# Turning the first mixer's residual with VectorE's block transposes and transfers

## The chip, the cores and the metric

The kernel runs on one core of a Trainium2 chip. Its metric is the device time in microseconds (us). The engines are TensorE (PE; its weight loads are listed as PEld), VectorE (DVE), ScalarE (ACT), GpSimd (POOL) and SyncE (SP), which issues all transfers. They run side by side and meet at semaphores.

## The reference

Attention over 8 heads with a local window and a few global keys gives `x` of 2 x 768 x 512 (batch, tokens, channels). Two mixers follow. The change lies in the first one:

```python
xt = x.transpose(0, 2, 1)
h = np.maximum(xt @ w_tok1, 0.0) @ w_tok2      # over tokens: 768 -> 256 -> 768
u = x + h.transpose(0, 2, 1)
h2 = np.maximum(u @ w_ch1, 0.0) @ w_ch2        # over channels: 512 -> 1536 -> 512
x = u + h2
```

The second mixer (angles, sine and cosine, token products, channel product) follows on its output. All is in fp32.

## The kernel before

Every fp32 matrix product is made of three products of parts: each operand is split into a rounded high part (`hi`, fp32r) and the rest (`lo`), and `three` (line 272 holds its matmul) issues hi x hi, hi x lo and lo x hi. The matmuls of both mixers up to the last channel product have this one line. ScalarE usually makes the high part, VectorE the low part; of the weights, GpSimd makes both (lines 573 and 574), chunk by chunk of 1536 columns, in one buffer pair `wraw` that SP fills (line 432).

Attention works in 48 steps (12 tiles of 128 tokens, 4 pairs of heads each). In a step VectorE takes the scores from PSUM (line 903), splits keys and queries of a later step (lines 810 and 799), and divides the weighed values into `act_raw`, where a tile lies with tokens on partitions (line 829). GpSimd splits queries (506) and, between them, the first two weight chunks. Eight more chunks follow behind the last tile of batch 0.

The first mixer, for each batch b: `hidden_tokens` gives 2 x 128 hidden units with the 512 channels as columns in banks 4 and 5; ScalarE and VectorE make high and low parts in `hid` (717, 1007). `mixed_tokens(s, j)` gives `h` for 128 tokens on partitions and 512 channels as columns, 6 tiles of 2 x 3 matmuls. VectorE adds the rows of `act_raw` into `u_rows` (1024), `turn_u` turns them on TensorE with four transposes into bank 4 or 5 (1243), and ScalarE (723) and VectorE (1016, from the bank) make the parts of the turned `u` in `split`, channels on partitions and tokens as columns. `hidden` and `reduce_hidden` then work in 24 blocks (2 halves of 384 tokens, 12 blocks of 128 hidden units), 12 matmuls each. In order: hidden 0, the last `turn_u`, hidden 1, reduce 0, hidden 2, reduce 1 and so on; the relu's parts are made by ScalarE (732) and VectorE (1034), and reduce i waits for the low part of block i.

The order of work on each engine is the order of its program, written out by hand; there is no planner. On VectorE the additions and low parts of `u` alternate, and the low part of hidden block 0 stands behind them. GpSimd's first chunk after attention waits for the last tile of batch 0 to be split (`tile_lo`), the chunk of the second mixer's first weights for all of `h` of batch 1 (`h_ready`). SP's list is: queries, keys and values of all tiles, two weight chunks between them, then the other weights, each behind `w_ready`, then the outputs.

Of the kernel before, what the change touches and what calls it, by code (L numbers as in the profile page):

```python
# [27 lines left out]
P = 128  # L28
# [42 lines left out]
HALF = 1024  # L71
BORROWED = 5
# [13 lines left out]
def build(nc, qk, v, both_counts, weights, out):  # L86
# [11 lines left out]
    with ctx:  # L98

        probs_mem = ExitStack()  # L100
# [4 lines left out]
        wraw = sb("wraw", [P, 2, CHUNK])  # L105
        act_raw = sb("act_raw", [P, B, DM * S // P])
# [56 lines left out]
        u_rows = sb("u_rows", [P, 2, DM], F32, mix1_mem)  # L163
# [55 lines left out]
        uT_ready = sem("uT_ready")  # L219
# [69 lines left out]

        def load_flag(eng):  # L290
            eng.wait_ge(flag_ready, 1)
            return eng.value_load(use_general[0:1, 0:1], min_val=0, max_val=1)

        def general_sync(sp, flag):
            with sp.If(flag > 0):
                sp.wait_ge(x_done, 2 * UNITS)
                for b, h, t, c in general_tiles(sp):
                    sp.wait_ge(gen_x, c + 1)
                    sp.dma_start(g_q[:, :], qk[b, bass.ds(t, 1), 0:D, bass.ds(h, 1), 0:P].rearrange(
                        "t d o s -> (t d) (o s)")).then_inc(gen_in, 16)  # L300
                    sp.dma_start(g_k[:, :].rearrange("d (t s) -> d t s", t=T),
                                 qk[b, :, 0:D, bass.ds(h, 1), P + G:].rearrange(
                                     "t d o s -> d t (o s)")).then_inc(gen_in, 16)
                    sp.dma_start(g_v[:, :, :], v[b, :, :, 0, bass.ds(h * VD, D)].rearrange(
                        "t s d -> s t d")).then_inc(gen_in, 16)

# [32 lines left out]
        def general_vector(dve, flag):  # L339
            with dve.If(flag > 0):  # L340
# [57 lines left out]
                dve.wait_ge(gen_x, B * H * T + 1)  # L398
                for g in range(AHEAD):
# [27 lines left out]
        def _(sp):  # L427
# [42 lines left out]
        def _(pool):  # L470
# [83 lines left out]
            for i in range(len(BESIDE), len(ORDER)):  # L554
# [33 lines left out]
        def _(act):  # L588
# [121 lines left out]
            for b in range(B):  # L710
# [8 lines left out]
                for s in range(T):  # L719
                    act.wait_ge(uT_ready, b * T + s + 1)  # L720
                    if b and s == 0:
                        act.wait_ge(x2_done, b * NC * KD)
                    act.activation(split[:, 0].rearrange("p (k s) -> p k s", k=KD)[:, :, s * P:(s + 1) * P],
                                   bank[4 + s % 2][:, :].rearrange("p (k s) -> p k s", k=KD),
                                   ACT.Copy).then_inc(uT_hi, 1)
# [44 lines left out]
        def _(dve):  # L770
# [101 lines left out]
            for m in range(STEPS):  # L872
# [119 lines left out]
            for b in range(B):  # L992
# [26 lines left out]
                for s in range(T):  # L1019
                    g = b * T + s  # L1020
                    dve.wait_ge(h_ready, g + 1)
                    if g >= 2:
                        dve.wait_ge(uT_ready, g - 1)
                    dve.tensor_tensor(u_rows[:, s % 2], bank[s % 4][:, :], raw[:, s * DM:(s + 1) * DM],
                                      ALU.add).then_inc(u_done, 1)
# [84 lines left out]
        def _(pe):  # L1110
# [79 lines left out]
            def hidden_tokens(b, s, j):  # L1190
# [3 lines left out]
                if b and s == 0:  # L1194
                    pe.wait_ge(uT_lo, b * T)
# [24 lines left out]
            for b in range(B):  # L1220
# [16 lines left out]
                def turn_u(s):  # L1237
                    g = b * T + s
                    pe.wait_ge(u_done, g + 1)
                    if g >= 2:  # L1240
# [6 lines left out]
                def mixed_tokens(s, j):  # L1247
                    g = b * T + s
                    pe.wait_ge(h1_lo, b * KJ + j + 1)
                    if j == 0 and s >= 4:  # L1250
                        pe.wait_ge(u_done, g - 3)
                    if b and j == 0 and s < 4:
                        pe.wait_ge(acc_taken, ((b * NC) - 1) * KD + s + 1)
                    return three(pe, bank[s % 4][:, :], lambda a: w_at(TOK2, a, j * S + s * P, P),
                                 lambda a: h1s[:, j, a], j == 0, j == KJ - 1)

                mixed_tokens(0, 0)
                mixed_tokens(1, 0)
                for s in range(T):
                    if s >= 2:  # L1260
                        mixed_tokens(s, 0)
                    mixed_tokens(s, 1).then_inc(h_ready, 1)
                    if s >= 2:
                        turn_u(s - 2)
                turn_u(T - 2)


                def hidden(i):
# [4 lines left out]
                    if f == 0:  # L1273
                        pe.wait_ge(uT_lo, b * T + (c + 1) * T // NC)
# [8 lines left out]
                def reduce_hidden(i):  # L1283
# [4 lines left out]
                    pe.wait_ge(r1_lo, g + 1)  # L1288
                    for d in range(KD):
# [8 lines left out]
                turn_u(T - 1)  # L1298
# [134 lines left out]
```

## Time and profile before

| | |
|---|---|
| median of 3 runs | 513.64 us (513.61 to 514.79) |
| the profiled execution's own time | 514.9 us |
| its span | 512.7 us |
| TensorE's share of the chain that ended last | 91% |
| share of it in the matmuls of line 272 | 72% |
| transfers | 37.20 MB, mean 73 GB/s |

The span is what the profile covers, from the first instruction to the last; the execution's own time also holds what lies around it. The chain is followed back from the last instruction to what released it at each step. A group's line number can be that of a helper (line 272), so the names of tiles tell which product it is.

### The profile page before, as it was taken

What the parts mean: (1) busy time and instruction counts of PE and PEld (TensorE: products, weight loads), DVE (VectorE), ACT (ScalarE), POOL (GpSimd) and SP (SyncE); (2) the same over time, 40 slices, a digit from 0 to 9 for tenths busy, and PEclk for the clock granted to TensorE, in tenths of its full rate; (3) what the DMA queues carried; (4) which work ended last, traced back from release to release, by engine and by line L of the source; (5) the groups of instructions that cost most, each with busy time, mean ns of one, the idle gap of its engine ahead of it and who ended that gap; (6) DMA issues with size and microseconds to landing.
All of it is one profiled execution on the core that took longest, in us unless ns stands there. A gap on an engine that the chain in (4) does not pass through costs nothing.

```text
span 512.7 us, 8107 instructions
## 1 busy us (share of the span) xinstructions
PE 504.5 (98%) x3049; PEld 471.1 (92%) x3049; DVE 258.8 (50%) x679; ACT 173.9 (34%) x371; POOL 144.2 (28%) x143
## 2 busy tenths in 40 slices
PE   7999999999999999999999999999999999999997
PEld 5899999879999999979999999998888899888897
DVE  7999998552111421164111424166775565754452
ACT  6899898521111111122111143413322320321130
POOL 4576766199900000005000041820310310000040
PEclk9999999999999999999999999999999999999999
DMA  5886675135410000003000011420000011000002
GB/s 195 310 301 233 221 264 160 45 123 150 137 42 1 0 2 0 1 0 99 28 0 1 0 63 61 124 83 0 1 1 2 0 63 61 1 1 0 1 31 93
DMA packets 9112, 37.20 MB, mean 73 GB/s; under 512 B 1136, under 2 KB 3184, under 8 KB 7664
## 3 DMA queue, kind: packets, MB, share of 16 engines
q1 hardware_dynamic: 9072, 36.67, 21.1%
q8 instruction: 25, 0.41, 0.3%
q14 instruction: 15, 0.12, 0.1%
HBM read 33.52 MB, written 3.15 MB: 72 GB/s over the span
## 4 chain that ended last, share of the span: by engine, by line
PE 91%; DMA 3%; DVE 2%; issue 1%; POOL 1%; ACT 1%; DVEq 0%; POOLq 0%; ACTq 0%
PE bank L272 72%; PE bank L1360 7%; PE bank L1125 3%; PE bank L1155 3%; PE bank L1158 2%; DMA qk_raw<-qk 2%; PE bank L1139 1%; PE bank L1137 1%; PE bank L1216 1%; PE bank L1243 1%; POOL wsplit L506 1%; DMA counts<-both_counts 1%; PE bank L1165 0%; DVE scores L903 0%; ACT bias L618 0%
## 5 line engine op out<-in xcount | busy, mean ns | idle before, releaser
L272 PE MATMUL bank<-hid,wsplit 128*128 128x384 f32 (+1 forms) x648 | 126.4, 344 | 0.1
L272 PEld LDWEIGHTS bank<-hid,wsplit 128*128 128x128 f32 x648 | 113.2, 188 | 4.0 <-issue 0.7
L272 PE MATMUL bank<-split,wsplit 128*128 128x384 f32 x576 | 108.1, 337 | 0.0
L272 PE MATMUL bank<-wsplit,zs 128*128 128x512 f32 (+1 forms) x576 | 104.1, 340 | 0.0
L272 PEld LDWEIGHTS bank<-wsplit,zs 128*128 128x128 f32 x576 | 89.1, 188 | 13.3
L272 PEld LDWEIGHTS bank<-split,wsplit 128*128 128x128 f32 x576 | 100.3, 188 | 0.0
L1034 DVE SCALAR_TENSOR_TENSOR hid<-bank,hid 128x384 fp32r<-128x384 f32 x48 | 26.7, 557 | 140.4 <-ACT hid L732 140.4
L574 POOL TENSOR_TENSOR wsplit<-wraw,wsplit 128x1536 fp32r<-128x1536 f32 (+1 forms) x18 | 58.7, 3263 | 75.5 <-ACT wsplit L693 74.5
L732 ACT ACTIVATE hid<-bank 128x384 fp32r<-128x384 f32 x48 | 23.6, 491 | 143.4 <-PE bank L272 143.4
L573 POOL CAST wsplit<-wraw 128x1536 fp32r<-128x1536 f32 (+1 forms) x12 | 15.9, 1328 | 136.1 <-PE bank L272 122.8
L506 POOL TENSOR_TENSOR wsplit<-qk_raw,wsplit 64x256 fp32r<-64x256 f32 x48 | 38.9, 810 | 26.5 <-DVE wsplit L810 24.8
L583 POOL TENSOR_TENSOR split<-act_raw,split 128x384 fp32r<-128x384 f32 x12 | 12.5, 1069 | 113.5 <-ACT split L766 113.5
L650 ACT ACTIVATE probs<-scores,nmax 128x232 f32<-128x232 f32 (+1 forms) x96 | 39.9, 465 | 2.4 <-DVE nmax L903 2.3
L697 ACT ACTIVATE zb<-zb 128x512 f32<-128x512 f32 x12 | 7.6, 632 | 96.1 <-DVE zb L976 96.1
L272 PE MATMUL bank<-wsplit,tile 128*128 128x512 f32 x144 | 35.5, 395 | 0.0
L1125 PE MATMUL bank<-wsplit 128*128 128x232 f32 (+1 forms) x192 | 32.7, 292 | 2.5 <-DVE wsplit L799 1.2
L1155 PE MATMUL bank<-vt,probsT 128*128 128x65 f32 x192 | 33.9, 265 | 0.9 <-ACT probsT L596 0.9
L1360 PE MATMUL bank<-split,wsplit 128*128 128x384 f32 x192 | 34.6, 341 | 0.0
L903 DVE CUSTOM_DVE_ANT_0 scores<-bank,bias 128x232 f32<-128x232 f32 (+1 forms) x96 | 32.4, 373 | 3.0 <-PE bank L1125 2.7
L1360 PEld LDWEIGHTS bank<-split,wsplit 128*128 128x128 f32 x192 | 33.8, 188 | 0.0
L272 PEld LDWEIGHTS bank<-wsplit,tile 128*128 128x128 f32 x144 | 26.4, 188 | 5.5
L1158 PE MATMUL bank<-vt,probsT 104*128 104x65 f32 x160 | 30.9, 275 | 0.0
(101 smaller groups left out, 583.3 us busy)
## 6 DMA issues: line engine op xcount, KB each, us to landing
wraw<-weights SPq DMA_DIRECT2D x16, 768.0 KB, 4.2
qk_raw<-qk SPq DMA_DIRECT2D x11, 1056.0 KB, 5.5
vt<-v SPq DMA_DIRECT2D x10, 520.0 KB, 5.2
out<-act_raw SPq DMA_DIRECT2D x16, 192.0 KB, 1.9
wraw<-weights SPq DMA_DIRECT2D x4, 512.0 KB, 3.5
qk_raw<-qk SPq DMA_DIRECT2D x2, 264.0 KB, 3.5
qk_raw<-qk SPq DMA_DIRECT2D x1, 528.0 KB, 6.0
vt<-v SPq DMA_DIRECT2D x2, 260.0 KB, 6.4
```

The lines of the kernel that those rows point to most:

```text
L272: mm = pe.matmul(dst, lhs(a), rhs(c), start=first and i == 0, stop=last and i == 2, skip_group_check=True)
L506: pool.tensor_tensor(q_split[D:P, n % 2, heads], q_in[D:P, n % 2, heads], q_split[D:P, n % 2, heads].bitcast(F32), ALU.subtract).then_inc( ...
L573: link(pool.tensor_copy(w_at(slot, 0, 0, width), raw))
L574: pool.tensor_tensor(w_at(slot, 1, 0, width), raw, w_at(slot, 0, 0, width).bitcast(F32), ALU.subtract).then_inc(w_ready, 1)
L650: act.activation(probs[:, n % 2, h, first:], scores[:, m % 2, e, first:], ACT.Exp, bias=nmax[:, n % 2, h:h + 1], scale=-1.0).then_inc(exp_ ...
L732: act.activation(r1s[:, i % 3, 0], bank[6 + i % 2][:, 0:SC], ACT.Relu).then_inc(r1_hi, 1)
L903: dve.tensor_tensor_reduce(out=scores[:, m % 2, e, first:], in0=S_BANK[m % 2][e][:, first:WIN], in1=bias[:, h, first:], scale=-SCALE, scal ...
L1034: dve.scalar_tensor_tensor(r1s[:, i % 3, 1], bank[6 + i % 2][:, 0:SC], 0.0, r1s[:, i % 3, 0].bitcast(F32), ALU.max, ALU.subtract).then_inc ...
L1125: mm = pe.matmul(S_BANK[m % 2][e][:, first:WIN], q_split[:, n % 2, h, :], k_split[:, i, h, key:key + WIN - first], start=i == 0, stop=i == 1)
L1155: mm = pe.matmul(dst, probsT[:, m % 2, at + P:at + 2 * P], vt[:, n % 2, 0, cols], start=m % 2 == 0 and e == 0, stop=n % T == 0, skip_group ...
L1158: mm = pe.matmul(dst, probsT[0:SEEN, m % 2, at:at + P], vt[0:SEEN, n % 2, 1, cols], start=False, stop=True, skip_group_check=True)
L1360: return pe.matmul(bank[at][:, 0:SC], w_at(CHAN_AT[k_ // 2], w, k_ % 2 * DM + d * P, P), S_(u, k_, c * SC, SC), start=first, stop=last, sk ...
```

## The change

The residual is turned ahead of time instead of `u` behind the product. VectorE's `transpose` of a 128 x 512 tile turns its 32 x 32 blocks in place; 16 transfers between partition groups of 32 then put the blocks where they belong, so that `xT` holds `x` with channels on partitions. Batch 0's six tiles are turned in attention's steps 26, 29, ..., 41 into `turned_early`, which lies in weight slots not yet in use; batch 1's in two sets of three, behind hidden blocks 3 to 5 and 9 to 11 of batch 0. SP issues batch 0's 16 transfers behind its last load of `v` and in front of the third weight chunk, batch 1's 2 x 16 behind weight chunk 11. GpSimd's third chunk waits for `xT_in` too.

`mixed_tokens(i, j)` now takes `hid` as the stationary operand and 384 columns of the weights as the moving one: 8 blocks of 128 channels x 384 tokens. VectorE adds `xT` from SBUF to the bank and writes `u` back into `xT`; ScalarE copies the high part out of `xT`, and VectorE's `lo_of_u` subtracts that from `xT`. `turn_u` is gone. Hidden 0 waits for four low parts (`uT_lo`), reduce 0 for all eight additions (`u_done`).

```diff
+        def move_quads(sp, src, first, count, done):
+            from_ = src.rearrange("p (t q c) -> p t q c", t=count, q=P // QUAD)
+            to = xT[:, first * DM:(first + count) * DM].rearrange("p (t a c) -> p t a c", t=count, a=P // QUAD)
+            for a in range(P // QUAD):
+                for q in range(P // QUAD):
+                    sp.dma_start(to[q * QUAD:(q + 1) * QUAD, :, a],
+                                 from_[a * QUAD:(a + 1) * QUAD, :, q]).then_inc(done, 16)
+
+        def turn_rows(dve, dst, b, t):
+            return dve.transpose(dst, act_raw[:, b, t * DM:(t + 1) * DM].rearrange(
+                "p (k q i) -> p q k i", k=KD, q=P // QUAD))
...
+            sp.wait_ge(x_turned, T)
+            move_quads(sp, turned_early[:, :], 0, T, xT_in)
             general_sync(sp, load_flag(sp))
             for i in range(len(BESIDE), len(ORDER)):
                 load_weight(i)
+                if i == SLOTS + 1:
+                    for first in range(0, T, STAGED):
+                        sp.wait_ge(x_turned, T + first + STAGED)
+                        move_quads(sp, turned[:, :], first, STAGED, xT_in)
...
                     pool.wait_ge(tile_lo, T)
+                    pool.wait_ge(xT_in, BATCH_IN)
                 if i == SLOTS + THETA:
-                    pool.wait_ge(h_ready, B * T)
+                    pool.wait_ge(h_ready, B * OUTB)
...
+                for i in range(OUTB):
+                    act.wait_ge(u_done, b * OUTB + i + 1)
...
+                    act.activation(by_quads(split[:, 0, u_cols(i)]), xT_at(i), ACT.Copy).then_inc(uT_hi, 1)
...
+                t, off = divmod(m - TURN_FROM, TURN_EVERY)
+                if 0 <= t < T and off == 0:
+                    dve.wait_ge(x_done, 2 * t + 2)
+                    turn_rows(dve, turned_early[:, t * DM:(t + 1) * DM], 0, t).then_inc(x_turned, 1)
...
-                def lo_of_uT(s):
-                    dve.wait_ge(uT_hi, b * T + s + 1)
-                    dve.tensor_tensor(rows_at(lo_, s), bank[4 + s % 2][:, :].rearrange("p (k s) -> p k s", k=KD),
-                                      rows_at(hi, s).bitcast(F32), ALU.subtract).then_inc(uT_lo, 1)
...
+                def lo_of_u(i):
+                    dve.wait_ge(uT_hi, b * OUTB + i + 1)
+                    dve.tensor_tensor(by_quads(lo_[:, u_cols(i)]), xT_at(i),
+                                      by_quads(hi[:, u_cols(i)].bitcast(F32)), ALU.subtract).then_inc(uT_lo, 1)
+
+                dve.wait_ge(xT_in, (2 * b + 1) * BATCH_IN)
+                for i in range(OUTB):
+                    dve.wait_ge(h_ready, b * OUTB + i + 1)
+                    dve.tensor_tensor(xT_at(i), by_quads(U_BANK[i][:, 0:SC]), xT_at(i),
                                       ALU.add).then_inc(u_done, 1)
-                    if s:
-                        lo_of_uT(s - 1)
-                lo_of_uT(T - 1)
-                dve.wait_ge(u_done, (b + 1) * T)
+                    if i:
+                        lo_of_u(i - 1)
+                lo_of_u(OUTB - 1)
...
+                    if b == 0 and 3 <= i < 3 + 2 * T and (i - 3) % T < STAGED:
+                        t = (i - 3) // T * STAGED + (i - 3) % T
+                        if t == STAGED:
+                            dve.wait_ge(xT_in, 2 * BATCH_IN)
+                        turn_rows(dve, turned[:, t % STAGED * DM:(t % STAGED + 1) * DM], b + 1,
+                                  t).then_inc(x_turned, 1)
...
-                def turn_u(s):
-                    g = b * T + s
-                    pe.wait_ge(u_done, g + 1)
-                    if g >= 2:
-                        pe.wait_ge(uT_lo, g - 1)
-                    for d in range(KD):
-                        mm = pe.transpose(bank[4 + s % 2][:, d * P:(d + 1) * P],
-                                          u_rows[:, s % 2, d * P:(d + 1) * P], ident[:, :])
-                    mm.then_inc(uT_ready, 1)
-
...
+                def mixed_tokens(i, j):
+                    c, k_ = divmod(i, KD)
                     pe.wait_ge(h1_lo, b * KJ + j + 1)
...
+                    if j == 0 and i in (6, 7):
+                        pe.wait_ge(u_done, b * OUTB + i - 5)
...
+                    return three(pe, U_BANK[i][:, 0:SC], lambda a: h1s[:, j, a, k_ * P:(k_ + 1) * P],
+                                 lambda a: w_at(TOK2, a, j * S + c * SC, SC), j == 0, j == KJ - 1)
+
+                for i in range(KD):
+                    mixed_tokens(i, 0)
+                for i in range(KD):
+                    mixed_tokens(i, 1).then_inc(h_ready, 1)
+                for i in range(KD, OUTB):
+                    mixed_tokens(i, 0)
+                    mixed_tokens(i, 1).then_inc(h_ready, 1)
...
                     if f == 0:
-                        pe.wait_ge(uT_lo, b * T + (c + 1) * T // NC)
+                        pe.wait_ge(uT_lo, b * OUTB + (c + 1) * KD)
...
                     pe.wait_ge(r1_lo, g + 1)
+                    if i == 0:
+                        pe.wait_ge(u_done, (b + 1) * OUTB)
```

## Rows read from the trace of the kernel before

**Rows 1.** The page, busy time, share of the span and instructions of the engines.
```profile
PE 504.5 (98%) x3049; PEld 471.1 (92%) x3049; DVE 258.8 (50%) x679; ACT 173.9 (34%) x371; POOL 144.2 (28%) x143
```

**Rows 2.** The chain of waits in time's order, batch 0's mix: start, us, what.
```profile
107.89 0.44 PE bank L1243 x4
108.33 1.40 PE bank L272 x6
...
112.04 0.61 ACT split L723
...
114.02 0.66 PE bank L1243 x4
114.67 2.12 PE bank L272 x12
```

**Rows 3.** Timeline, both mixes: start, us, engine, line, operation, tiles, count, idle before.
```profile
103.46 4.44 PE L272 MATMUL bank<-hid,wsplit 128*128 128x512 f32 x18
...
119.20 1.98 PE L272 MATMUL bank<-hid,wsplit 128*128 128x384 f32 x10
...
223.64 4.48 PE L272 MATMUL bank<-hid,wsplit 128*128 128x512 f32 x18
...
239.39 1.79 PE L272 MATMUL bank<-hid,wsplit 128*128 128x384 f32 x9
```

**Rows 4.** Windows: stretch, length, each engine's busy time, TensorE's clock, transfers.
```profile
7.00:9.00 2.00, 0.83 (x5) 0.40 (x4) 1.86 (x7) 1.49 (x7) 0.73 (x1) 1.00 0.99 410
...
54.00:60.00 6.00, 5.49 (x50) 5.37 (x49) 5.97 (x28) 4.78 (x15) 4.63 (x7) 1.00 0.78 272
...
66.00:72.00 6.00, 6.00 (x56) 6.00 (x56) 5.70 (x30) 5.92 (x16) 4.68 (x8) 1.00 0.74 263
```

**Rows 5.** Timeline, attention.
```profile
1.45 5.16 PE L1165 MATMUL bank<-wsplit 128*128 128x512 f32 x13 [1.45 <-DVE wsplit L779]
...
59.09 0.68 PE L1125 MATMUL bank<-wsplit 128*128 128x232 f32 x4 [0.52 <-DVE nmax L903]
...
63.05 0.52 POOL L533 CAST wsplit<-wraw 128x256 fp32r<-128x256 f32 x1
...
63.32 0.54 DVE L799 TENSOR_TENSOR wsplit<-qk_raw,wsplit 128x272 fp32r<-128x272 f32 x1
```

**Rows 6.** Timeline, GpSimd's weights beside batch 0's mix.
```profile
100.70 1.47 POOL L573 CAST wsplit<-wraw 128x1536 fp32r<-128x1536 f32 x1 [13.28 <-DVE third L860]
...
102.25 3.51 POOL L574 TENSOR_TENSOR wsplit<-wraw,wsplit 128x1536 fp32r<-128x1536 f32 x1
...
105.71 1.47 POOL L573 CAST wsplit<-wraw 128x1536 fp32r<-128x1536 f32 x1
```

**Rows 7.** Timeline, VectorE on two SBUF tiles of 384 columns, GpSimd idle.
```profile
341.66 1.96 DVE L957 TENSOR_TENSOR act_raw<-act_raw,split 128x384 f32<-128x384 f32 x4
```

**Rows 8.** Timeline, VectorE beside a subtraction of GpSimd in the second mixer.
```profile
358.20 0.69 DVE L984 TENSOR_TENSOR zc<-bank,zc 128x512 f32<-128x512 f32 x1 [1.31 <-ACT zc L698]
...
359.00 2.41 POOL L574 TENSOR_TENSOR wsplit<-wraw,wsplit 128x1024 fp32r<-128x1024 f32 x1
...
359.59 2.37 DVE L989 TENSOR_TENSOR zs<-zc,zs 128x512 fp32r<-128x512 f32 x1
...
361.88 0.68 DVE L989 TENSOR_TENSOR zs<-zb,zs 128x512 fp32r<-128x512 f32 x1
```

**Rows 9.** Timeline, GpSimd at the end of batch 1's mix.
```profile
233.77 1.04 POOL L573 CAST wsplit<-wraw 128x1024 fp32r<-128x1024 f32 x1 [93.06 <-PE bank L272]
```

**Rows 10.** Timeline, SP at the end of attention.
```profile
82.41 0.33 SPq L455 DMA_DIRECT2D vt<-v  x1
83.79 3.98 SPq L432 DMA_DIRECT2D wraw<-weights  x2
```

**Rows 11.** The page, transfers: tiles, queue, count, KB each, us to landing.
```profile
wraw<-weights SPq DMA_DIRECT2D x16, 768.0 KB, 4.2
...
out<-act_raw SPq DMA_DIRECT2D x16, 192.0 KB, 1.9
```

More of the change, by code:

```diff
@@ L71 @@
 HALF = 1024
+QUAD = 32
+TURN_FROM = 26
+TURN_EVERY = 3
+STAGED = 3
+BATCH_IN = 16 * 16
 BORROWED = 5
@@ L98, in build @@
     with ctx:
+        turned_mem = ExitStack()
+        sb("below_turned", [P, CH1, 2, CHUNK], F32, turned_mem)
+        turned_early = sb("turned_early", [P, T * DM], F32, turned_mem)
+        turned_mem.close()
         probs_mem = ExitStack()
@@ L105, in build @@
         wraw = sb("wraw", [P, 2, CHUNK])
+        xT = sb("xT", [P, DM * S // P])
         act_raw = sb("act_raw", [P, B, DM * S // P])
@@ L162, in build @@
         zc = sb("zc", [P, DM])
-        u_rows = sb("u_rows", [P, 2, DM], F32, mix1_mem)
+        turned = sb("turned", [P, STAGED * DM], F32, mix1_mem)
         hid = sb("hid", [P, 2 * 3 * SC], F32R, mix1_mem)
@@ L218, in build @@
         u_done = sem("u_done")
-        uT_ready = sem("uT_ready")
+        x_turned = sem("x_turned")
+        xT_in = sem("xT_in")
+        gen_turned = sem("gen_turned")
+        gen_xT = sem("gen_xT")
         uT_hi = sem("uT_hi")
@@ L284, in build, with xT_at, by_quads, u_cols @@
         U2_DVE = [(0, d) for d in range(2, KD)]
+        U_BANK = [bank[0], bank[1], bank[2], bank[3], bank[4], bank[5], bank[0], bank[1]]
+        def xT_at(i):
+            c, k_ = divmod(i, KD)
+            groups = SC // QUAD
+            return xT[:, :].rearrange("p (w k j) -> p k w j", k=KD, j=QUAD)[:, k_, c * groups:(c + 1) * groups]
+        def by_quads(ap):
+            return ap.rearrange("p (w j) -> p w j", j=QUAD)
+        def u_cols(i):
+            c, k_ = divmod(i, KD)
+            return slice(k_ * S + c * SC, k_ * S + (c + 1) * SC)
+        def move_quads(sp, src, first, count, done):
[8 more added lines that the diff above has]
+                "p (k q i) -> p q k i", k=KD, q=P // QUAD))
         def load_flag(eng):
@@ L305, in general_sync @@
                         "t s d -> s t d")).then_inc(gen_in, 16)
+                sp.wait_ge(gen_turned, T)
+                move_quads(sp, turned_early[:, :], 0, T, gen_xT)
         def general_pool(pool, flag):
@@ L398, in general_vector @@
                 dve.wait_ge(gen_x, B * H * T + 1)
+                dve.wait_ge(xT_in, BATCH_IN)
+                for t in range(T):
+                    turn_rows(dve, turned_early[:, t * DM:(t + 1) * DM], 0, t).then_inc(gen_turned, 1)
+                dve.wait_ge(gen_xT, BATCH_IN)
                 for g in range(AHEAD):
@@ L717, in _ @@
                     act.activation(h1s[:, j, 0], bank[4 + j][:, :], ACT.Relu).then_inc(h1_hi, 1)
-                for s in range(T):
-                    act.wait_ge(uT_ready, b * T + s + 1)
-                    if b and s == 0:
+                for i in range(OUTB):
+                    act.wait_ge(u_done, b * OUTB + i + 1)
+                    if b and i == 0:
                         act.wait_ge(x2_done, b * NC * KD)
-                    act.activation(split[:, 0].rearrange("p (k s) -> p k s", k=KD)[:, :, s * P:(s + 1) * P],
-                                   bank[4 + s % 2][:, :].rearrange("p (k s) -> p k s", k=KD),
-                                   ACT.Copy).then_inc(uT_hi, 1)
+                    act.activation(by_quads(split[:, 0, u_cols(i)]), xT_at(i), ACT.Copy).then_inc(uT_hi, 1)
                 for i in range(CHB):
@@ L1194, in hidden_tokens @@
                 if b and s == 0:
-                    pe.wait_ge(uT_lo, b * T)
+                    pe.wait_ge(u_done, b * OUTB)
                 return three(pe, bank[4 + j][:, :], lambda a: w_at(TOK1, a, s * F_TOK + j * P, P),
@@ L1257, in _ @@
[L1257 to L1265, printed above, removed]
+                def mixed_tokens(i, j):
+                    c, k_ = divmod(i, KD)
+                    pe.wait_ge(h1_lo, b * KJ + j + 1)
+                    if j == 0 and i in (4, 5):
+                        pe.wait_ge(h1_lo, (b + 1) * KJ)
+                    if j == 0 and i in (6, 7):
+                        pe.wait_ge(u_done, b * OUTB + i - 5)
+                    if b and j == 0 and i < KD:
+                        pe.wait_ge(acc_taken, ((b * NC) - 1) * KD + i + 1)
+                    return three(pe, U_BANK[i][:, 0:SC], lambda a: h1s[:, j, a, k_ * P:(k_ + 1) * P],
+                                 lambda a: w_at(TOK2, a, j * S + c * SC, SC), j == 0, j == KJ - 1)
@@ L1297, in _ @@
                 hidden(0)
-                turn_u(T - 1)
                 for i in range(1, CHB):
@@ L1425 @@
     }
-    nc = bacc.Bacc("TRN2", target_bir_lowering=False, num_devices=1)
+    nc = bacc.Bacc("TRN2", target_bir_lowering=False, num_devices=1,
+                   dynamic_dma_scratch_size=1024)
     args = [nc.dram_tensor(n, a.shape, mybir.dt.from_np(a.dtype), kind="ExternalInput").ap()
```

14 lines of the change are left out of this document (removed).

## The prediction

> **What bounds the kernel now.** First the page: TensorE is busy 98% of the span, VectorE half of it, GpSimd 28% [rows 1]. Then the chain of waits in order of time: behind attention it is TensorE's own matmuls, with short breaks [rows 2]. So a change pays only by taking work or a break from TensorE, and costs only where another engine makes TensorE wait. In the token mixer the chain shows what could go: groups of four transposes at 0.44 us, and one visit to ScalarE, an issue and VectorE before the next group. The same stretch as a timeline gives its length: the second token product starts at 103.46 and the first product that needs `hid` again at 119.20, 15.74 us; in batch 1 223.64 to 239.39, 15.75 [rows 3]. I call these two stretches the mixes. Next I read who is near its limit beside TensorE: in attention VectorE is busy 5.97 of 6 us in the stretch from 54 [rows 4] and once makes TensorE wait 0.52 [rows 5]; GpSimd works without a break from 100.70, splitting eight chunks of weights [rows 6], which is exactly while batch 0's mix runs.
>
> **TensorE's own sum.** Removed: 12 groups of transposes, 12 x 0.44 = 5.3 us, 2.65 a mix. The token product keeps its columns: before 36 matmuls of 512, after 48 of 384. Six of 512 take 1.40 (0.233 each), twelve of 384 take 2.12 (0.177 each) [rows 2]; 8.40 becomes 8.50. Two hidden products are 24 x 0.177 = 4.25. Before: 8.40 + 2.65 + 4.25 = 15.3, so 0.44 of the 15.74 is breaks, and the chain's 112.04 to 114.02 is where they stand. After, if nothing is late: 8.50 + 4.25 = 12.75, 2.99 less a mix, 6.0 in all. This is what the edit can give.
>
> **Who feeds the hidden product now.** Per 384-column block VectorE adds the residual and later subtracts ScalarE's rounded copy. Before, both operations read one PSUM operand; now the add reads PSUM and `xT`, but the subtraction (`lo_of_u`) reads `xT` and `split`, both in SBUF. An operation of 384 columns of either kind takes 0.55 and follows the last after 0.49 (four in 1.96) [rows 7], so a block costs VectorE 0.98 and TensorE 6 x 0.177 = 1.06. Undisturbed, the fourth subtraction ends some 0.9 us before TensorE finishes block 8: no wait, and `xT` is ready as below.
>
> **GpSimd beside it.** A VectorE operation with two SBUF inputs does not run beside GpSimd's. At 359.00 GpSimd starts a subtraction of 2.41 us; VectorE's add from PSUM at 358.20, beside GpSimd's cast, takes its usual 0.69, but the subtraction of two SBUF tiles at 359.59, otherwise 0.69, takes 2.37, to 0.55 past GpSimd's end; the next starts at 361.88, 0.47 past it [rows 8]. The pair of rows comes once more in the trace, a tile later, and attention has the same on a small scale. GpSimd's casts hold VectorE too: one from 63.05 to 63.57, and a VectorE subtraction with two SBUF inputs that starts inside it at 63.32 ends at 63.86 [rows 5]. So VectorE waits for the GpSimd instruction in progress and goes before the next. GpSimd alternates 1.55 (cast) and 3.46 us (subtraction), start to start [rows 6].
> The Trainium skill, SBUF — State Buffer, section "SBUF: two separate sides", says it as an exclusive lock held for a whole instruction, also for two SBUF inputs against a GpSimd operation that reads SBUF. It adds what no row shows, that an operation with one SBUF input outside the two-port modes is free of it; by that the six new transposes are not stopped, and the sum below has nothing for them; if they were, each would wait for up to one GpSimd slice, and the attention term would go towards its upper bound.
>
> **Batch 0, step by step** (clock of the profile before). Mix starts 103.46; blocks are ready at 106.1, 106.6, 107.2, 107.7, then each 1.06 later. Add 0 at 106.4; ScalarE's copy ends 107.5; subtraction 0 is asked at 107.5 and waits for GpSimd's 107.25-110.7. Then add 2, subtraction 1 waits for the cast (till 112.6), add 3, subtraction 2 waits for the next 3.46 (till 116.6), add 4, subtraction 3 till 118.5. It alternates: subtractions 4 to 7 start at 122.4, 124.4, 128.3, 130.3. A pair takes 1.5 + 3.5 + twice 0.47. TensorE has ended its 48 matmuls at 111.97, waits for subtraction 3 until 119.3, does hidden 0 and 1 to 123.5, and then waits again: VectorE makes the low part of hidden 0 only behind subtraction 7, at 131.2, so the reduction starts at 131.4. Before it started at 119.20: 12.2 us lost. Shifting GpSimd's phase by -1.5 to +4.5 us in the same steps gives 9.7 to 12.2; if subtraction 7 keeps its place right behind 6, 1.4 less.
> TensorE's clock: granted 1.00, and its longest break is the 1.2 us in the stretch from 7 to 9 [rows 4]; now it idles 7 and 8 us. The kernel's first 13 matmuls of 512 columns, after idling, took 5.16 us [rows 5]; at 0.233 each 13 take 3.03 [rows 2]. I charge one such start, 2.1 us, behind the second wait (the first one's is covered). Bounds 0 and 4.2.
> The Trainium skill, TensorE: Matmul & The Clock Gate, Part 1, says that an idle engine returns to half of 2.4 GHz, which is the direction of this term; that the granted clock reads 1.00 in those first microseconds as well is not explained by it.
>
> **Batch 1.** GpSimd idles 93 us until all of `h` is done and then, from 233.77, runs 1.04 [rows 9], 2.41 [rows 8] and both once more. Subtractions 0 to 4 or 5 are through; two or three are held, the reduction starts at 238.0 to 238.9 instead of 236.4. Against 239.39 this is 0.5 to 1.4 gained; I take 1.4 (bounds 0.5 and 3.0).
>
> **Attention.** Six transposes of 128x512 are added to VectorE. No row shows one; the nearest is a 512-column VectorE operation, 0.69 [rows 8]; below it stands 0.49, the pace of 384 columns [rows 7], above it twice 0.69, if the blocks went through in two passes. The first stands at step 26, near 56 us, where VectorE has no idle time [rows 4] and TensorE already waits for it [rows 5]: 0.65 in full. The other five add 3.45 in the next 27 us, of which VectorE's idle 0.3 in 6 us (5.70 busy, from 66) takes back 1.3 [rows 4]. The 2.1 left are a lag, and two sets of scores cover one step of it (16 matmuls of 56 in 6 us, 1.7 us [rows 4]): some 0.5 reaches TensorE. I take 1.2. Bounds: 0, if the buffers take all, and 6 x 0.69 = 4.1.
> The Trainium skill, VectorE: DVE Perf Modes, section "The three transpose paths", gives 311 ns for 128x128 in bf16 on VectorE; four make 1.24 us by estimate, nearly twice my 0.69, and would make the attention term about 4 us.
>
> **SP, the transfers and the weights.** On SP weight 2 is issued at 83.79, right behind the last load of `v` [rows 10]. The 16 moves go ahead of it. An issue takes 0.33 [rows 10]: 5.3 us of SP, so weight 2 starts near 89. A transfer of 768 KB lands in 4.2, one of 192 KB in 1.9 [rows 11]; 16 moves of 98 KB at the first's rate end near 93, all one behind the other at 1.9 each at 114. I take 96. GpSimd first needs `xT` at 100.70 [rows 6], VectorE at 106.4 as above, and GpSimd weight 2 at 100.70, so this costs nothing; if late, GpSimd's chain shifts, which is in the phases above. Weight 2 is split by 105.7 [rows 6] and used at 114.67 [rows 2], the next one five later and at 119.20 [rows 3]: 8.5 us of cover, and the need comes later now. Batch 1's transposes and moves stand at hidden blocks 3 to 5 and 9 to 11, 4.25 us each with 1.1 us of VectorE work, on a queue with no load due: nothing. Should GpSimd stop such a transpose for 3.5 us, the next low part would be 0.5 late against some 0.8 of cover.
>
> **Sum.** +12.2 + 2.1 - 1.4 + 1.2 = +14.1 us. The profiled execution has a span of 512.7 and its own time is 514.9, 1.3 above the median 513.64. It would take 529.0; against the median 527.7.
>
> **Rivals.**
> (a) No hold-up in the mixes (faster). If VectorE's subtractions slip through, the change gives its 6.0 less 1.2 of attention: 508.8. For it: the sum of matmuls is certain. Against it: the stretched operations of rows 8. It decides at one place, the duration of `lo_of_u` beside GpSimd: 0.55 or up to 4. Undisturbed, the reduction would start at 116.2; from 3 us of holds on, less than one GpSimd subtraction, batch 0's mix is slower than before, and from 8 us on the whole kernel.
> (b) GpSimd goes first after each of its instructions. As it has no gaps, subtraction 0 waits for the end of the eighth chunk, 100.7 + 8 x 5.0 = 140.7; seven more blocks follow, the reduction starts near 149: about 545. Against it: in rows 8 VectorE goes on right behind GpSimd, though there GpSimd had nothing next.
> (c) Moves at 1.9 us each: `xT` at 114, first add 7.6 us later, then the same alternation: 535. For it: pieces of 32 partitions that no row shows. Against it: 768 KB that land in 4.2 [rows 11].
>
> **Chances.** Forecast 0.80, its own range 521 to 534 (phase and slot -3.9, clock -2.1 and +2.1, attention -1.2 and +2.9, batch 1 -1.6 and +0.9; not all on one side). (a) 0.12, (b) 0.03, (c) 0.05. Were casts no hindrance and only GpSimd's subtractions held VectorE, a pair would take 5.5 instead of 5.9 us and the result would stay in this range. The range 517 to 536 leaves out (a), (b) and some of the forecast's own edges. A change of 0.3% (1.5 us) is about what can be told from none. Faster: (a), 0.11; within: 0.01 of (a) and 0.01 of the forecast; slower: 0.87.
>
> **What would show it.** Right: in batch 0's mix `split<-xT,split` on VectorE with a mean of 2 to 3 us, each ending 0.55 after a GpSimd instruction, and TensorE waiting about 7 and 8 us for VectorE; the same operation at 0.55 in batch 1's first blocks; TensorE waits in attention of about 1 us in all. Wrong: `lo_of_u` at 0.55 throughout in batch 0, or a transpose that takes well over 0.7, or GpSimd waiting for a transfer beyond 100.70.

## The result, and the profile after

The changed kernel takes 526.99 us (median of 6 runs, 524.45 to 528.58); the kernel before took 514.7 in the same session (513.61 to 515.26). The ratio is 1.024, interval 1.021 to 1.027: slower, as forecast (527.7). The two profiled executions compared below have spans of 526.8 and 512.7 us, so 14.1 us have to be found.

The page of the changed kernel: busy time of the engines, and two lines of the span in 40 slices.

```profile
PE 506.8 (96%) x3025; PEld 476.6 (90%) x3025; DVE 282.1 (54%) x699; ACT 175.1 (33%) x375; POOL 147.0 (28%) x143
...
PE   8999999955999999999999999999999999999997
...
PEclk9999999997899999999999999999999999999999
```

Against [rows 1] TensorE has 24 instructions fewer but is busy 2.3 us longer (a slower clock, below), and VectorE is busy 23.3 us longer for 20 instructions more. The slices put the place at the ninth and tenth, 105 to 132 us, batch 0's first mixer. The matmuls of line 285 are those of line 272 before. TensorE's waits, all of them in us, times, longest:

```profile
PE bank L285 <- DVE split L1070: 6.4, 1, 6.4
PE bank L285 <- DVE hid L1085: 6.1, 2, 5.2
```

VectorE in batch 0's mix (start, us, engine, line, operation, tiles, shape, count). L1076 adds `xT` to the bank, L1070 is `lo_of_u`:

```profile
107.36 1.02 DVE L1076 TENSOR_TENSOR xT<-bank,xT 128x384 f32<-128x384 f32 x2 [1.73 <-PE bank L285]
108.52 3.62 DVE L1070 TENSOR_TENSOR split<-xT,split 128x384 fp32r<-128x384 f32 x1
112.06 0.54 DVE L1076 TENSOR_TENSOR xT<-bank,xT 128x384 f32<-128x384 f32 x1
112.53 1.35 DVE L1070 TENSOR_TENSOR split<-xT,split 128x384 fp32r<-128x384 f32 x1
113.80 0.55 DVE L1076 TENSOR_TENSOR xT<-bank,xT 128x384 f32<-128x384 f32 x1
114.27 3.31 DVE L1070 TENSOR_TENSOR split<-xT,split 128x384 fp32r<-128x384 f32 x1
...
125.17 5.06 DVE L1070 TENSOR_TENSOR split<-xT,split 128x384 fp32r<-128x384 f32 x2
130.16 1.01 DVE L1085 SCALAR_TENSOR_TENSOR hid<-bank,hid 128x384 fp32r<-128x384 f32 x2
```

The pair from 125.17 in the view of its tile, over that stretch alone (ns, shortest, median, longest, then the first and last start):

```profile
L1070 DVE TENSOR_TENSOR split<-xT,split x2: 1812/2570/3327, 125.2 to 128.4; 128x384 fp32r<-128x384 f32 x2
```

GpSimd beside it:

```profile
108.22 3.51 POOL L626 TENSOR_TENSOR wsplit<-wraw,wsplit 128x1536 fp32r<-128x1536 f32 x1
111.66 1.81 POOL L625 CAST wsplit<-wraw 128x1536 fp32r<-128x1536 f32 x1
113.55 3.61 POOL L626 TENSOR_TENSOR wsplit<-wraw,wsplit 128x1536 fp32r<-128x1536 f32 x1
117.11 1.79 POOL L625 CAST wsplit<-wraw 128x1536 fp32r<-128x1536 f32 x1
...
128.03 1.79 POOL L625 CAST wsplit<-wraw 128x1536 fp32r<-128x1536 f32 x1
```

Two things show here. The addition, with one operand in PSUM, keeps 0.54 us; it starts at 112.06 beside GpSimd's cast and is not held. The subtractions, with both in SBUF, end at 112.14, 113.88 and 117.58, each 0.41 or 0.42 behind the end of the GpSimd instruction beside it (111.73, 113.47, 117.16). And the hold works both ways: GpSimd's cast, 1.47 us before [rows 6], takes 1.81 where a VectorE subtraction goes first. The two engines alternate, one instruction each, even where VectorE has no addition between: of the last two subtractions the first (3.33) waits for GpSimd's subtraction and the second (1.81) for its cast at 128.03. TensorE over the same stretch:

```profile
104.37 8.71 PE L285 MATMUL bank<-wsplit,hid 128*128 128x384 f32 x48
119.46 6.17 PE L285 MATMUL bank<-split,wsplit 128*128 128x384 f32 x24 [6.38 <-DVE split L1070]
130.80 4.18 PE L285 MATMUL bank<-hid,wsplit 128*128 128x384 f32 x12 [5.18 <-DVE hid L1085]
134.78 3.26 PE L285 MATMUL bank<-split,wsplit 128*128 128x384 f32 x12
137.88 2.28 PE L285 MATMUL bank<-hid,wsplit 128*128 128x384 f32 x12
```

The clock in windows (stretch, length, busy time and count of PE, PEld, DVE, ACT, POOL, then the granted clock, transfers):

```profile
116.00:119.40 3.40, 0.00 (x0) 0.00 (x0) 3.40 (x4) 0.53 (x1) 3.32 (x3) 0.57 0.37 103
119.40:126.00 6.60, 6.17 (x24) 5.88 (x24) 6.60 (x6) 1.77 (x4) 6.52 (x3) 0.71 0.51 183
...
130.80:134.00 3.20, 3.20 (x10) 3.20 (x11) 0.36 (x1) 0.00 (x0) 3.20 (x2) 0.50 0.17 71
134.00:137.80 3.80, 3.80 (x16) 3.80 (x15) 0.00 (x0) 0.00 (x0) 3.72 (x2) 0.61 0.65 211
137.80:141.00 3.20, 3.20 (x20) 3.20 (x19) 0.56 (x1) 0.49 (x1) 3.12 (x3) 1.00 0.45 137
```

Behind each stop TensorE runs at 0.50, the 1.2 GHz level, and returns to 1.00 while it works. In windows of 0.2 us the granted clock is 0.50 from 116.5 to 123.3, and again from 130.1 to 136.9; of the first of these stretches 3.8 us lie behind the restart at 119.46, of the second 6.1 us behind the restart at 130.80.

Batch 1's mix, where GpSimd comes late (TensorE, then VectorE, then GpSimd):

```profile
239.82 8.74 PE L285 MATMUL bank<-wsplit,hid 128*128 128x384 f32 x48
248.40 4.40 PE L285 MATMUL bank<-split,wsplit 128*128 128x384 f32 x24
253.73 2.37 PE L285 MATMUL bank<-hid,wsplit 128*128 128x384 f32 x12 [0.93 <-DVE hid L1085]
```
```profile
248.66 0.55 DVE L1070 TENSOR_TENSOR split<-xT,split 128x384 fp32r<-128x384 f32 x1
...
249.59 3.61 DVE L1070 TENSOR_TENSOR split<-xT,split 128x384 fp32r<-128x384 f32 x2
```
```profile
248.70 1.42 POOL L625 CAST wsplit<-wraw 128x1024 fp32r<-128x1024 f32 x1 [105.20 <-PE bank L285]
250.20 2.59 POOL L626 TENSOR_TENSOR wsplit<-wraw,wsplit 128x1024 fp32r<-128x1024 f32 x1
```

The same `lo_of_u` takes 0.55 while GpSimd idles, and the last two of eight are held together.

The moves and transposes (from the page, KB each and us to landing; from the tile's own view, ns min/median/max; from SP's timeline):

```profile
xT<-turned_early SPq DMA_DIRECT2D x16, 96.0 KB, 2.6
```
```profile
L322 SPq DMA_DIRECT2D xT<-turned_early x16: 590/614/872, 83.7 to 94.1; - x16
L326 DVE STREAM_TRANSPOSE turned_early<-act_raw x6: 697/698/704, 56.3 to 82.7; 128x512 f32<-128x512 f32 x6
```
```profile
83.70 11.03 SPq L322 DMA_DIRECT2D xT<-turned_early  x16
96.42 0.81 SPq L477 DMA_DIRECT2D wraw<-weights  x2
```

Where the 14.1 us are, from these rows and [rows 3]:

| stretch | before | after | difference |
|---|---|---|---|
| start of the kernel to batch 0's mix | 103.46 | 104.37 | +0.9 |
| batch 0's mix to its first reduction | 15.74 | 26.43 | +10.7 |
| that reduction to batch 1's mix | 104.44 | 109.02 | +4.6 |
| batch 1's mix to its first reduction | 15.75 | 13.91 | -1.8 |
| the rest | 273.3 | 273.1 | -0.2 |

The third line has two parts. The first 24 matmuls of 384 columns after the second stop take 7.08 us (130.80 to 137.88); at the pace of the blocks before, 4.16 for 24, that is +2.9. The remaining +1.7 I had no cause for: 21 later blocks take 4.24 us each instead of 4.16. VectorE's low part of the relu comes once a block and shows it, before and after:

```profile
140.80 0.56 DVE L1034 SCALAR_TENSOR_TENSOR hid<-bank,hid 128x384 fp32r<-128x384 f32 x1 [3.60 <-ACT hid L732]
144.96 0.56 DVE L1034 SCALAR_TENSOR_TENSOR hid<-bank,hid 128x384 fp32r<-128x384 f32 x1 [3.60 <-ACT hid L732]
```
```profile
147.09 0.56 DVE L1085 SCALAR_TENSOR_TENSOR hid<-bank,hid 128x384 fp32r<-128x384 f32 x1 [3.07 <-ACT hid L782]
...
151.32 0.56 DVE L1085 SCALAR_TENSOR_TENSOR hid<-bank,hid 128x384 fp32r<-128x384 f32 x1 [3.06 <-ACT hid L782]
```

The starts are 4.16 and then 4.23 apart, with the granted clock at 1.00 in both. In batch 1 the changed kernel is back at 4.16 behind its stop of 0.93.

### The profile page after: what moved, and what is told of

Read it like the earlier page. It is cut to its first block, busy times and chain, and to the rows that moved or that the text cites. A ratio compares the mean times of both kernels' runs of the same rounds, so it can differ in the third digit from the quotient of the medians.

```text
span 526.8 us, 8116 instructions
## 1 busy us (share of the span) xinstructions
PE 506.8 (96%) x3025; PEld 476.6 (90%) x3025; DVE 282.1 (54%) x699; ACT 175.1 (33%) x375; POOL 147.0 (28%) x143
## 4 chain that ended last, share of the span: by engine, by line
PE 86%; DVE 8%; DMA 3%; POOL 1%; ACT 1%; issue 1%; DVEq 0%; POOLq 0%; ACTq 0%
PE bank L285 67%; PE bank L1408 6%; DVE split L1070 5%; PE bank L1182 3%; PE bank L1212 3%; PE bank L1215 2%; DMA qk_raw<-qk 2%; PE bank L1196 1%; DVE xT L1076 1%; PE bank L1194 1%; PE bank L1273 1%; POOL wsplit L557 1%; DMA counts<-both_counts 1%; PE bank L1222 0%; ACT bias L670 0%
## 5 line engine op out<-in xcount | busy, mean ns | idle before, releaser
L285 PE MATMUL bank<-split,wsplit 128*128 128x384 f32 x576 | 111.2, 344 | 6.4 <-DVE split L1070 6.4
L285 PE MATMUL bank<-hid,wsplit 128*128 128x384 f32 x576 | 110.4, 342 | 6.1 <-DVE hid L1085 6.1
L285 PEld LDWEIGHTS bank<-split,wsplit 128*128 128x128 f32 x576 | 104.2, 193 | 6.7 <-issue 6.7
L285 PEld LDWEIGHTS bank<-hid,wsplit 128*128 128x128 f32 x576 | 102.9, 191 | 6.8 <-issue 5.5
L625 POOL CAST wsplit<-wraw 128x1536 fp32r<-128x1536 f32 (+1 forms) x12 | 17.9, 1493 | 146.8 <-PE bank L285 134.3
L1408 PE MATMUL bank<-split,wsplit 128*128 128x384 f32 x192 | 34.3, 339 | 0.0
L1408 PEld LDWEIGHTS bank<-split,wsplit 128*128 128x128 f32 x192 | 33.5, 188 | 0.0
```

The costliest lines, as they stand in the source:

```text
L285: mm = pe.matmul(dst, lhs(a), rhs(c), start=first and i == 0, stop=last and i == 2, skip_group_check=True)
L1408: return pe.matmul(bank[at][:, 0:SC], w_at(CHAN_AT[k_ // 2], w, k_ % 2 * DM + d * P, P), S_(u, k_, c * SC, SC), start=first, stop=last, sk ...
```

## The experiments

By the prediction two facts together make the hold-up: `lo_of_u` has two operands in SBUF, and GpSimd works at the same time. The first two runs take away one each. The rival is that something else (the idle itself, the moves, the transposes) makes the time. Each run's time is a median with its own median of the kernel before; ratios have their 95% interval.

**u_in_bank.** The sum is written back to the bank, and ScalarE and VectorE read it there; GpSimd is left as it is.

```diff
-  dve.tensor_tensor(xT_at(i), by_quads(U_BANK[i][:, 0:SC]), xT_at(i), ALU.add)
+  dve.tensor_tensor(by_quads(U_BANK[i][:, 0:SC]), by_quads(U_BANK[i][:, 0:SC]), xT_at(i), ALU.add)
   # lo_of_u and ScalarE's copy: xT_at(i) -> by_quads(U_BANK[i][:, 0:SC])
   # TensorE's three waits for u_done -> the same counts of uT_lo
```

> The changed kernel, but VectorE's addition writes u back into its PSUM bank (ScalarE's copy and VectorE's subtraction read the bank), so the subtraction has one SBUF input as before the change. Theory (GpSimd's weight instructions hold VectorE's operations with two SBUF inputs): subtractions take 0.55 us in batch 0 as well, the mix falls from 26.4 to about 12.8 us, TensorE never idles there, no slow clock: about 527 - 13.7 (mix) - 4.6 (clock and pace behind it) - 1 (batch 1) = 508 us against 514.7 before. Rival (the subtraction is slow for its access pattern, or because the transfers into xT are late): it stays stretched or the first addition stays late, 520 us or more.

Measured: 512.2 us against 514.55, ratio 0.995 (0.994 to 0.997). VectorE, then GpSimd:

```profile
108.44 0.56 DVE L1071 TENSOR_TENSOR split<-bank,split 128x384 fp32r<-128x384 f32 x1
```
```profile
108.16 3.51 POOL L626 TENSOR_TENSOR wsplit<-wraw,wsplit 128x1536 fp32r<-128x1536 f32 x1
111.62 1.46 POOL L625 CAST wsplit<-wraw 128x1536 fp32r<-128x1536 f32 x1
```

Beside the same GpSimd subtraction the operation now takes 0.55 instead of 3.62, GpSimd's cast is back at 1.46, and neither mix has a stop. The sum kept in PSUM, where VectorE's subtraction and with it ScalarE's copy read it, is worth 14.8 us against the changed kernel (526.99 to 512.2). It misses the expected 508 by 4: all blocks of batch 0 and the first 17 of batch 1 now take 4.24 us, 40 x 0.08 = 3.2 us; the last six of batch 1 take 4.16.

**gpsimd_behind.** `lo_of_u` is left in SBUF, and GpSimd's fourth chunk waits until batch 0's eight low parts are done.

```diff
+                if i == len(BESIDE) + 1:
+                    pool.wait_ge(uT_lo, OUTB)
```

> The changed kernel, but GpSimd waits with its fourth weight chunk until all eight low parts of u of batch 0 are made. Theory: no GpSimd instruction beside the subtractions, so they take 0.55 us with two SBUF inputs too; hidden 0 and 1 end near 117 us; the fourth chunk is ready 5 us behind the last low part, near 121, and the reduction starts there instead of at 130.8: about 9.6 us less, and with the short idle time little or none of the 4.6 us behind it: 513 to 517. Rival (transfers or access pattern): the reduction starts no earlier than at 131 plus what the late chunk costs, 527 or more.

Measured: 515.73 against 514.55, ratio 1.004 (1.002 to 1.005). VectorE, GpSimd and TensorE:

```profile
107.45 0.56 DVE L1072 TENSOR_TENSOR split<-xT,split 128x384 fp32r<-128x384 f32 x1
```
```profile
114.43 1.47 POOL L627 CAST wsplit<-wraw 128x1536 fp32r<-128x1536 f32 x1 [8.77 <-DVE split L1072]
```
```profile
111.87 4.40 PE L285 MATMUL bank<-split,wsplit 128*128 128x384 f32 x24
119.45 3.92 PE L285 MATMUL bank<-hid,wsplit 128*128 128x384 f32 x12 [3.19 <-POOL wsplit L628]
```

So two SBUF operands alone cost nothing (0.56); it is the pair that costs. The stop comes back smaller, as a wait for weights of 3.2 us, and in batch 1, where the wait does not apply, the last two subtractions are held as in the changed kernel.

**before_idle** asks what an idle TensorE costs by itself: the kernel before, with a wait for the seventh weight chunk (not needed there) ahead of hidden 0. One run.

```diff
+                if b == 0:
+                    pe.wait_ge(w_ready, 7)
                 hidden(0)
```

> The kernel before, with nothing of the change, but in batch 0 TensorE waits in front of hidden 0 until GpSimd has made chunk 6, from 114.4 to 125.7 us: an idle time of 11.3 us alone. If the 2.9 us behind the changed kernel's second wait and the blocks of 4.24 instead of 4.16 us for the rest of batch 0 come from TensorE's idle time: granted clock near 0.5 for some us, blocks of 4.24 until batch 1, 514.7 + 11.3 + 2 to 3 + 1.7 = 530 us. If the slower blocks belong to the change (transfers, VectorE's transposes, the swapped operands): blocks of 4.16, 528 us. If neither: 526 us.

Measured: 526.72 us, span 524.5, 11.8 more than before's. TensorE:

```profile
124.71 3.92 PE L272 MATMUL bank<-split,wsplit 128*128 128x384 f32 x12 [10.87 <-POOL wsplit L574]
```

The stop is 10.9 and the first 12 matmuls behind it take 3.76 us start to start (to the next instruction at 128.47) instead of 2.12 [rows 2]: 1.6 for the clock, at a mean granted clock of 0.53. The changed kernel lost 2.9 behind its second stop. The granted clock tells why more: here it is 0.50 for 3.5 us behind the restart (124.71 to 128.2), there for 6.1 (130.80 to 136.9), and half of each is about what was lost. By its trace this is the expectation's case of 528. The time is lower because the stop and the clock's cost are shorter than the 11.3 and 2 to 3 us put in there, and because the mix starts at 102.63, 0.8 earlier than in the kernel before. Blocks stay at 4.16, so a stop does not by itself bring the pace of 4.24.

**bank_late_turns**: u_in_bank with `TURN_FROM = 30`, away from the stretch where VectorE has no idle time [rows 4].

> As the kernel with u in the bank, and the six transposes of batch 0 stand at steps 30 to 45 instead of 26 to 41. Theory: the 0.9 us that attention lost comes from the first transpose, where TensorE waits for VectorE; at step 30 and later the buffers cover it, so attention ends 0.5 to 0.9 us earlier: about 507.5 us. The 16 moves then end near 101 us, 6 us before the first addition; the third weight chunk arrives 1 to 2 us late at GpSimd, with 8 us of cover. Rival: each transpose costs TensorE alike wherever it stands: no difference. Other rival: the moves or the chunk come too late: 0.5 us or more slower.

Measured: 512.25, ratio 0.995 (0.994 to 0.997), the same as u_in_bank. The mix starts at 105.17, no earlier than u_in_bank's 104.32, and in batch 0's blocks VectorE waits 5.97 us for the first set of batch 1's moves (153.2 to 159.1); behind that the blocks take 4.16. Where the transposes stand in attention does not matter to what can be measured.

**before_turns**: the kernel before with only the six transposes added at steps 26 to 41, into memory that nobody reads.

> The kernel before, with the six transposes of batch 0 added at steps 26 to 41 and nothing else of the change (no moves, their result unused). Theory: this is the attention term of the sum, some 0.9 to 1.2 us more than before, 515.6. If the moves and not the transposes delay the end of attention: no difference to before, 514.6.

Measured: 515.01 against 514.64, ratio 1.001 (1.000 to 1.002). The added work costs 0.4 us, which can't be told from nothing, where I had charged 1.2.

**bank_tail_turns**: u_in_bank with the transposes at steps 42 to 47 and weight chunks 3 and 4 issued in front of the moves.

> The kernel with u in the bank, the six transposes of batch 0 at steps 42 to 47, where VectorE has less to do, and SP issues weight chunks 3 and 4 ahead of the 16 moves. Theory (the transposes cost only where VectorE is at its limit): attention as before the change, 0.9 us less than with them at 26 to 41, 511.3; the moves land near 104 us, ahead of the first addition at 106.4. Rival: the moves come later than the first addition, or GpSimd's late start makes the fourth chunk late at the first reduction (2.5 us of cover): 512.5 or more.

Measured: 511.46, ratio 0.994 (0.992 to 0.996). That is near the 511.3 of the theory, but not for its reason: the mix starts at 104.44, so nothing is gained in attention, and GpSimd starts late, for the transfers:

```profile
105.95 1.47 POOL L627 CAST wsplit<-wraw 128x1536 fp32r<-128x1536 f32 x1 [17.30 <-DMA xT<-turned_early]
```

The weights come 4.3 us later than in the changed kernel (101.68) and TensorE still doesn't wait for them. What it gains on u_in_bank comes from the blocks of batch 0 that go over to 4.16 us from about 160 us on.

The next four runs ask what sets the pace of 4.16 or 4.24. All are u_in_bank with one edit, which acts ahead of hidden 0 of each batch.

**bank_wait6**: hidden 0 waits for six low parts instead of four, which makes a short stop.

```diff
-  pe.wait_ge(uT_lo, b * OUTB + (c + 1) * KD)
+  pe.wait_ge(uT_lo, b * OUTB + (OUTB if c else 6))
```

> The kernel with u in the bank, and hidden 0 waits for six low parts of u instead of four, so that TensorE has to stop for some 0.8 us behind the token product. What is open: the blocks of the channel products take 4.24 us there and 4.16 in the kernel before, with the same matmuls at the full clock. Theory A (the matmul stream has two steady paces and a stop of TensorE resets it to the quicker one): blocks of 4.16 in both batches, 2 x (24 x 0.08 - 0.8) = 2.2 us less, 510.0. Theory B (the pace belongs to what the change puts beside or ahead, as the transfers or the swapped operands): blocks of 4.24 and 1.6 us more, 513.8.

Measured: 511.0, ratio 0.993 (0.991 to 0.995). The time lies between the two that the theories gave. The stops are 0.75 and 0.66 us long; behind the first the blocks take 4.16, behind the second 4.24. A stop may change the pace but need not.

**bank_one_turn**: one needless transpose of the identity into a free bank.

```diff
+                pe.transpose(bank[7][:, 0:P], ident[:, :], ident[:, :])
                 hidden(0)
```

> The kernel with u in the bank, and one transpose of the identity on TensorE (0.11 us) in front of hidden 0, its result unused. Theory A in the form that the transposes between the products, which the change removed, set the pace: blocks of 4.16, 2 x (1.9 - 0.1) = 3.6 us less, 508.6. If only a stop sets it, and also by theory B: blocks of 4.24, 512.4.

Measured: 509.09 us (508.58 to 510.12), ratio 0.990 (0.987 to 0.992). TensorE in batch 0; the same in batch 1 from 229.32:

```profile
112.10 0.27 PE L1347 MATMUL bank<-ident 128*128 128x128 f32 x1
...
116.38 2.24 PE L285 MATMUL bank<-hid,wsplit 128*128 128x384 f32 x12
118.45 2.24 PE L285 MATMUL bank<-split,wsplit 128*128 128x384 f32 x12
```

In u_in_bank two such groups, here those of batch 1, start 2.12 us apart:

```profile
236.10 2.28 PE L285 MATMUL bank<-hid,wsplit 128*128 128x384 f32 x12
238.22 2.28 PE L285 MATMUL bank<-split,wsplit 128*128 128x384 f32 x12
```

With the added transpose it is 2.07 above and 2.09 in batch 1 (233.59 to 235.68). With that the first mixer of batch 0, from its mix to batch 1's, takes 117.19 us (103.55 to 220.74) instead of 118.96 (104.32 to 223.28), and an added instruction makes the kernel 3 us faster. Of the 3.3 us between the two profiled spans (510.3 and 507.0) 0.8 lie ahead of the mix, where the two kernels do the same work, so that some 2.5 are left for the pace.

**bank_two_turns** (two such transposes) and **bank_one_matmul** (a plain matmul of 384 columns) ask whether the number or the kind of the instruction matters.

```diff
+                for _ in range(2):
+                    pe.transpose(bank[7][:, 0:P], ident[:, :], ident[:, :])
```
```diff
+                    if i == 0:
+                        pe.matmul(bank[7][:, 0:SC], S_(0, 0, 0, P), S_(0, 0, 0, SC),
+                                  start=True, stop=True, skip_group_check=True)
```

> u_in_bank with two needless 128x128 transposes of the identity ahead of hidden product 0, instead of the one of bank_one_turn (509.1 us, blocks of 4.16 us in both batches). Theory A, any transpose behind the token product resets TensorE's pace to 173.3 ns per matmul of 384 columns: blocks of 4.16 us in both batches, about 509.5 us. Theory B, an extra instruction toggles between the two paces (an odd number of them turns it, an even number leaves it): blocks of 4.24 us in both batches as in u_in_bank, about 512.5 us.

> u_in_bank with one needless plain matmul of 384 columns (split's first tile, into a bank that is free) ahead of hidden product 0, where bank_one_turn has a transpose. Theory A, the reset is the transpose's: blocks of 4.24 us in both batches, about 512.4 us. Theory B, one more instruction of any kind turns the pace: blocks of 4.16 us in both batches, about 509.3 us.

Measured: 509.73 (ratio 0.990, 0.988 to 0.992) and 509.57 (0.992, 0.989 to 0.994), blocks of 4.16 us from hidden 0 on in both batches of both. So it is neither a toggle, which two would have undone, nor the transpose: Theory A of the first expectation fits, Theory A of the second falls. One or two instructions of another kind or operand between the token product and hidden 0 are enough here. The same kernels also show that the kind of instruction does not decide the pace. Behind the 17th reduction of batch 1 all of them have 12 other matmuls of 512 columns and a group of four transposes, and then six more blocks. Across that place the pace goes from 4.24 to 4.16 us in u_in_bank, bank_wait6 and bank_tail_turns, from 4.16 to 4.24 in bank_one_turn and bank_two_turns, stays at 4.24 in bank_late_turns and at 4.16 in bank_one_matmul. What in TensorE makes the two paces stays open; the three runs with an added instruction also move the first reduction against the start of the mix, by 0.03 to 0.13 us (12.80 in u_in_bank, 12.83, 12.93 and 12.90 here), and no run holds that still.

bank_one_turn beats both kernels: 1.0% under the kernel before, and 3.3% under the changed one by the two ratios (0.990 / 1.024). In it TensorE is busy 99% of a span of 507.0 us.

## Why the prediction was right

The forecast was 527.7, the result 526.99; the profiled execution took 528.58 for the 529.0 worked out against it. By its own steps:

- **TensorE's own sum** held. Without hold-up and with blocks of 4.16 us, the mixes of bank_one_turn take 12.83 (103.55 to 116.38) and 12.85 us (220.74 to 233.59), for 12.75 predicted; 5.8 us of the mixes are saved instead of 6.0. In the changed kernel itself this gain is there and covered. Rival (a)'s 508.8 is about what bank_one_turn reaches with its 509.09. So at the quick pace the rival's price was right; its condition, not its sum, was what failed.
- **GpSimd beside it** was the cause. u_in_bank and gpsimd_behind each take one half of the pair away and the stretched operations go. The length is as read from [rows 8]: 3.3 to 3.6 us behind GpSimd's subtraction and 1.35 behind its cast, ending 0.41 behind it, where the rows of before had 0.47 and 0.55. That VectorE goes before GpSimd's next instruction held as well; rival (b) had said no.
- **Batch 0 step by step**: 10.7 lost for 12.2 predicted. The mis-sized term is the pair, 1.5 + 3.5 + twice 0.47 = 5.94; it measures 5.45 (111.66 to 117.11), since VectorE's operation delays GpSimd's cast by 0.34 but its subtraction by only 0.10 (3.61 for 3.51). Three pairs lie between the ends of subtraction 0 and of subtraction 6 (112.14 to 128.50, 16.4 us), which is the 1.5 us. Subtraction 7 did not keep its place right behind 6, a cast went between, as I had taken it. TensorE's two stops were 6.4 and 5.2 us for about 7 and 8, and the mean of the eight `lo_of_u` was 2.43 us, for 2 to 3.
- **The clock**: 2.9 for 2.1. I charged one slow start of 13 matmuls of 512 columns, 5.16 us; the records show a granted clock of 0.50 from the restart at 130.80 to 136.9, some 6.1 us and 18 matmuls. The first stop's slow stretch was covered, as predicted: 24 matmuls in 6.17 us ended at 125.63, while VectorE's low part came at 130.2 or later.
- **Batch 1**: -1.8 for -1.4, within its bounds. Two subtractions were held, the mildest of the cases given there.
- **Attention**: the mix starts 0.9 later for 1.2 predicted, but this is no proof. With the six transposes at these steps it starts between 103.31 and 104.62 in eight profiled executions of this study (mean 104.07), without them at 103.46 and 102.63, and before_turns puts their price at 0.4 us of the whole time. A 128x512 transpose takes 0.698, for my 0.69; the estimate of 1.24 that I had worked out from the Trainium skill's VectorE: DVE Perf Modes, "The three transpose paths", did not fit a tile of this shape. That GpSimd does not stop these transposes, with their one SBUF input, held: the one at 56.26 takes 0.70 beside a subtraction of GpSimd from 56.12 to 56.94.
- **SP, the transfers and the weights** cost nothing, as predicted, but the working was off. A move of 32-partition pieces keeps SP 0.61 us (the median; 0.87 at most) and the 16 together 11.0, not 0.33 and 5.3. Weight 2 is issued at 96.42, not near 89; the chunk it brings is needed at 119.46, and GpSimd's third chunk starts at 101.68, when VectorE has split the last tile. At the 4.2 us to landing of [rows 11] weight 2 is there near 100.6, an estimate, so that about 1 us of slack was left on this path. The landing of 2.6 us a move is above rival (c)'s 1.9, but they overlap, and so (c) does not follow.
- **Missing** in the sum: the pace of 4.24 us a block, +1.7. It and the 0.8 of the clock make up for the 1.5, 0.4 and 0.3 that batch 0, batch 1 and attention took less; the total is nearer than its terms are, and that closeness is luck.

## What to carry to other kernels

Before an operand is moved from PSUM to SBUF on VectorE, look who else works on SBUF in those microseconds: here a subtraction of 0.55 us became 3.6 beside GpSimd, and writing the intermediate back to the bank took all of that away with the order of work as it was. A sum of TensorE's columns tells what a change can give, and the last engine in front of the reduction tells whether it does. Where long runs of equal matmuls fill the time, compare their start-to-start spacing before and after, not only their count: 2% of it was 1.8 us in one batch here.

## What was not expected of the hardware

- Matmuls of 384 columns run at one of two steady paces with the granted clock at 1.00: 12 in 2.08 or in 2.12 us. One or two needless instructions ahead of hidden 0 bring the quick pace behind them in both batches (three runs of three), a short stop in one of two; but other instructions between blocks, late in batch 1, turn the quick pace into the slow one in two of these three runs. The cause is open.
- The hold between VectorE and GpSimd slows GpSimd too: casts of 1.47 us take 1.8, and four chunks that would take 5.0 each take 5.45 (111.66 to 133.50). The two take turns, one instruction each, where both have work ready, and VectorE's own next instruction does not go first (125.17 to 130.2, and in batch 1 249.59 to 253.2).
- SP takes 0.61 us to issue a transfer of 32-partition pieces of 96 KB, nearly twice the 0.33 of a load of `v` [rows 10].
